# One transpose for a tile's raw queries and keys, with GpSimd splitting them after the turn

## The chip, the cores and the metric

The kernel runs on one core of a Trainium2 chip. The metric is the device time of one execution in microseconds (us). Times of one kernel agree within about 0.03% here (999.93 to 1000.2 us in three runs).

## The reference

Attention with a threshold, then a mixture of experts, then a small network:

```python
scores = scale * q @ k.T                          # 4 x 8 heads, 576 rows, 64 columns, fp32
thresh = max(scores, rows) - tau
attn   = exp(where(scores >= thresh, scores, -1e9) - max)
x      = (attn / (sum(attn) + 1e-9)) @ v          # -> 2304 tokens x 512
x      = gate * relu(x @ w1[expert]) @ w2[expert] # one of 8 experts per token
out    = (h * sigmoid(1.702 h)) @ w_out, h = x @ w_in
```

## The kernel before

Each product of fp32 numbers is made of products of parts in the type float32r: a number is split into a high part (a copy into the type) and a low part (the number less the high part). For the scores, the 64 columns of a head fill only half of the 128 rows of TensorE's array, so the high and low parts of the queries lie one above the other (high in the upper 64 partitions, low in the lower 64) and are multiplied by the keys' parts in the same order and, in a second pass, in the swapped order (`k_swap`). The two passes give all four products.

**Pairs and steps.** Two heads of the same number in two batches make a pair. There are 16 pairs. Their 2 x 576 rows are turned as nine tiles of 128 rows: tiles 0 to 3 are rows of the first head (side 0), tile 4 has the last 64 rows of both, tiles 5 to 8 are the second head (side 1). So a pair has nine steps, u = 0 to 8 (`U`), two pairs make a quad (18 steps, i), and n counts steps over all pairs. Quad 0 is written out, quads 1 to 3 (pairs 2 to 7) are a rolled loop (`Fori`), quads 4 to 7 are written out again (`over_quads`), as other work is set between their steps. Each engine has its own program of the same steps. Nothing but semaphores orders them.

**What the engines do in step n of pair p:**
- TensorE: five transposes of the probabilities of step n - 5 (L1520), and between them the transposes of a tile of the *next* pair (L1534: one for the queries' parts, one for the keys'), both into banks of `pt_ps`; then `score(n)` (L1563: four matmuls of 288 columns, eight in step 4, whose tile belongs to both sides) into one of two buffers `s_ps`. In steps 1 and 5 `values` (L1577, 20 matmuls) of the pair before, in steps 3 and 7 `turn` (L1594 to L1602).
- VectorE: L1091 scales the scores into SBUF and takes the row's minimum (`row_low`); L811 writes results in steps 4 and 8; L802 masks the probabilities of step n - 2 with the threshold.
- GpSimd: L712 makes the threshold of the row from its minimum. Between the thresholds: in step 0 `split(pair + 1, 1)` and in step 5 `split(pair + 2, 0)` (L651 copy, L653 subtract, on the raw tiles `qk` with rows in partitions, into `qk_parts`); in step 1 `swap(pair, j, 1)` and in step 6 `swap(pair + 1, 1 - j, 0)` (L661, L663: two copies of 64 partitions x 576 from `qkT` to `k_swap`, each from one half of the partitions to the other).
- ScalarE: copies the turned probabilities to `pT` (L1302, L1307) and the turned queries and keys to `qkT` (L1315, in step 4 L1311 to L1313), then takes exp of the scores of step n - 1 (L1386). In steps 2 and 6 it copies the values' result (L1371).
- SyncE: loads the next pairs' queries, keys and values (`load_a`, `load_b`, `load_v`) and stores x; `load_a` and `load_b` wait until the split has read the buffer (`parts_ready`).

**The waits around the change.** `score` in step 0 waits for the swap of side 0, in step 4 for that of side 1:

```python
if u == 0:
    wait(pe, k_swapped, (quad * 2 + j) * 4 + 2)
if u == TAIL:
    wait(pe, k_swapped, (quad * 2 + j) * 4 + 4)
...
wait(pe, low_ready, n - 1)
```

The transposes of tile 0 and of tile 5 wait for their side's split. GpSimd takes its instructions in the order of its program, and each threshold waits for L1091 of its step.

After the attention come a mixture of experts on tiles of 256 tokens and the last network. GpSimd gathers the first two blocks of tokens for them in quad 7 (steps i = 3 and 11), and the first expert's weights are loaded to where `qk` lies.

Of the kernel before, what the change touches and what calls it, by code (L numbers as in the profile page):

```python
# [6 lines left out]
ALU = mybir.AluOpType  # L7
# [9 lines left out]
P = 128  # L17


def attention_moe_mlp_kernel(nc, q, k, v, tau, modality_id, w_gate, modality_bias, w1, w2, w_in, w_out, out):  # L20
# [54 lines left out]
    with ctx:  # L75
# [27 lines left out]
        qk = put("qk", [P, U, 2, DH], at=DB * F1)  # L103
        qk_parts = put("qk_parts", [P, U, 2, 2, DH], F32R)
# [3 lines left out]
        qkT = [put(f"qkT{b}", [P, 2, 2 * SPAD], F32R) for b in range(2)]  # L108
# [156 lines left out]
        first_a = [s_ps[0][:, c] for c in range(2)]  # L265
        first_t = [s_ps[1][:, c, 0:P] for c in range(2)]
        first_b = [pt_ps[:, 0:TAIL].rearrange("p a n -> p (a n)"), misc[:]]
# [13 lines left out]
        qk_a_loaded = sem("qk_a_loaded")  # L281
        qk_b_loaded = sem("qk_b_loaded")
        v_loaded = [sem(f"v_loaded{b}") for b in range(2)]
        k_swapped = sem("k_swapped")
        first_parts = sem("first_parts")
# [121 lines left out]

        A_ROWS, T_ROWS, B_ROWS = slice(0, TAIL), slice(TAIL, TAIL + 1), slice(TAIL + 1, U)
# [31 lines left out]
        def _(sp):  # L440
# [6 lines left out]
            def load_a(quad, j):  # L447

                if on(quad, 1, QUADS) or j == 1:
                    if isinstance(quad, int) and quad == 0:  # L450
                        sp.wait_ge(first_parts, 2)
                    else:
                        wait_apart(sp, parts_ready, (quad * 2 + j) * 4 - 4)
                for c, src in enumerate((q_v, k_v)):
                    one, two = seqs_of(src, quad, j)
                    sp.dma_start(qk[:, A_ROWS, c], one[0:SEQ - LAST].rearrange("(t p) d -> p t d", p=P)).then_inc(qk_a_loaded, 16)
                    sp.dma_start(qk[0:LAST, TAIL, c], one[SEQ - LAST:]).then_inc(qk_a_loaded, 16)
                for c, src in enumerate((q_v, k_v)):
                    one, two = seqs_of(src, quad, j)
                    sp.dma_start(qk[LAST:P, TAIL, c], two[SEQ - LAST:]).then_inc(qk_a_loaded, 16)  # L460

            def load_b(quad, j):

                wait_apart(sp, parts_ready, (quad * 2 + j) * 4 - 2)
                one, two = seqs_of(q_v, quad, j)
                for units, at in B_QUERIES:
                    sp.dma_start(qk[:, units, 0], two[at].rearrange("(t p) d -> p t d", p=P)).then_inc(qk_b_loaded, 16)
                one, two = seqs_of(k_v, quad, j)
                sp.dma_start(qk[:, B_ROWS, 1], two[0:SEQ - LAST].rearrange("(t p) d -> p t d", p=P)).then_inc(qk_b_loaded, 16)
# [32 lines left out]
            def load_w1(expert, turn):  # L502
                for a in range(DB):
# [26 lines left out]
            def early_part(quad, j):  # L530
# [6 lines left out]
                if (quad, j) == (QUADS - 2, 1):  # L537
                    sp.wait_ge(first_expert_ready, 1)
                    load_w1(sp.value_load(first_expert_i[0:1], min_val=0, max_val=E - 1), 0)
                if (quad, j) == (QUADS - 1, 1):  # L540
                    sp.wait_ge(turned, UNITS)
                    sp.wait_ge(order_stored, 16)
                    load_w2(sp.value_load(first_expert_i[0:1], min_val=0, max_val=E - 1), 0)

            def step(quad):
                for j in range(2):
                    pair = quad * 2 + j
                    if isinstance(quad, int):
                        early_part(quad, j)
                    if on(pair, 0, PAIRS):  # L550
                        load_v(quad, j)
                    if on(pair, 2, PAIRS + 2):
                        store_x(quad - 1, j)
                    if on(pair, 0, PAIRS - 2):
                        load_b(quad + 1, j)
                    if on(pair, 0, PAIRS - 3):
                        load_a(quad + 1 + j, 1 - j)

            sp.dma_start(qk[:, A_ROWS, 0], q_v[0, 0:SEQ - LAST].rearrange("(t p) d -> p t d", p=P)).then_inc(qk_a_loaded, 16)
# [1275 lines left out]
```

## Time and profile before

| | |
|---|---|
| median of 3 runs | 999.98 us |
| profiled execution | 1000.17 us, span 998.6 us |
| attention stage | from the first score at 11.02 us to about 335 us |
| TensorE busy in the span | 972.2 us (97%) |
| VectorE, ScalarE, GpSimd | 502.7, 447.3, 256.2 us |
| TensorE's mean granted clock | 0.995 |
| chain that ended last | TensorE 92%, VectorE 3% |

Busy time is the union of an engine's instructions. TensorE's matmuls overlap in it, so what one costs is read from the chain of waits, where pieces follow each other. The span is shorter than the execution's own time by 1.57 us.

### The profile page before, as it was taken

What the parts mean: (1) busy time and instruction counts of PE and PEld (TensorE: products, weight loads), DVE (VectorE), ACT (ScalarE), POOL (GpSimd) and SP (SyncE); (2) the same over time, 40 slices, a digit from 0 to 9 for tenths busy, and PEclk for the clock granted to TensorE, in tenths of its full rate; (3) what the DMA queues carried; (4) which work ended last, traced back from release to release, by engine and by line L of the source; (5) the groups of instructions that cost most, each with busy time, mean ns of one, the idle gap of its engine ahead of it and who ended that gap; (6) DMA issues with size and microseconds to landing.
All of it is one profiled execution on the core that took longest, in us unless ns stands there. A gap on an engine that the chain in (4) does not pass through costs nothing.

```text
span 998.6 us, 18965 instructions
## 1 busy us (share of the span) xinstructions
PE 972.2 (97%) x6508; PEld 867.1 (87%) x6509; DVE 502.7 (50%) x1142; ACT 447.3 (45%) x1013; POOL 256.2 (26%) x357
## 2 busy tenths in 40 slices
PE   5999999999999999999999999999999999999996
PEld 5778787878787799999999999989999999999995
DVE  6988788888889685212125155522223223222221
ACT  4778787878788514221124154422222222222221
POOL 5655565556565212111112100010010100100101
PEclk8999999999999999999999999999999999999999
DMA  3323222222344118511112542200100101000000
GB/s 62 73 60 72 47 60 65 66 49 61 91 103 130 38 42 255 178 42 42 42 42 79 173 159 64 64 32 1 32 32 0 56 7 32 32 0 0 32 1 32
DMA packets 106904, 61.08 MB, mean 61 GB/s; under 512 B 87373, under 2 KB 95587, under 8 KB 106851
## 3 DMA queue, kind: packets, MB, share of 16 engines
q1 hardware_dynamic: 96195, 44.36, 16.9%
q0 software_dynamic: 4160, 10.51, 3.4%
q10 hardware_dynamic: 6496, 5.54, 1.7%
q8 instruction: 28, 0.46, 0.2%
q14 instruction: 25, 0.20, 0.1%
HBM read 45.68 MB, written 14.70 MB: 60 GB/s over the span
## 4 chain that ended last, share of the span: by engine, by line
PE 92%; DVE 3%; issue 2%; ACT 1%; POOL 1%; DMA 0%; SPq 0%; ACTq 0%; POOLq 0%; DVEq 0%
PE s_ps L1790 20%; PE s_ps L1762 13%; PE s_ps L1628 11%; PE o_ps L1577 9%; PE pt_ps L1520 9%; PE s_ps L1563 8%; PE pt_ps L1762 6%; PE misc L1710 5%; PE o_ps L1710 5%; PE pt_ps L1534 3%; PE misc L1602 1%; PE pt_ps L1620 1%; PE misc L1594 1%; DMA qk<-in_k_dram 0%; ACT probs L1386 0%
## 5 line engine op out<-in xcount | busy, mean ns | idle before, releaser
L1279 DVE TENSOR_TENSOR g<-s_ps,sig 128x384 f32<-128x384 f32 x96 | 53.5, 557 | 277.1 <-ACT sig L1491 277.1
L1491 ACT ACTIVATE sig<-s_ps 128x384 f32<-128x384 f32 x96 | 47.2, 492 | 271.5 <-PE s_ps L1790 271.5
L1091 DVE TENSOR_SCALAR_CACHE_REDUCE scores<-s_ps,taus 128x576 f32<-128x576 f32 x144 | 117.7, 817 | 47.5 <-PE s_ps L1563 30.2
L802 DVE SCALAR_TENSOR_TENSOR probs<-scores,thresh,probs 128x576 f32<-128x576 f32 x144 | 136.6, 950 | 0.0
L1520 PE MATMUL pt_ps<-ident,probs 128*128 128x128 f32 x720 | 127.0, 278 | 3.9 <-ACT pT L1302 1.8
L1790 PE MATMUL s_ps<-yT_high,w_in_high 128*128 (+1 forms) x384 | 129.5, 337 | 0.3 <-issue 0.2
L1790 PE MATMUL s_ps<-yT_high,w_in_low 128*128 (+1 forms) x384 | 129.5, 337 | 0.0
L1790 PE MATMUL s_ps<-yT_low,w_in_high 128*128 (+1 forms) x384 | 128.9, 336 | 0.0
L757 POOL DMA_INDIRECT out_dram<-out_sb,table x18 | 17.8, 989 | 417.7 <-ACT out_sb L1466 414.7
L1386 ACT ACTIVATE probs<-scores,row_low 128x576 f32<-128x576 f32 x144 | 115.4, 801 | 7.5 <-DVE scores L1091 6.1
L1520 PEld LDWEIGHTS pt_ps<-ident,probs 128*128 128x128 f32 x720 | 83.5, 141 | 28.0 <-issue 18.4
L712 POOL TENSOR_TENSOR thresh<-row_low,taus 128x1 f32<-128x1 f32 x144 | 74.1, 515 | 121.4 <-DVE scores L1091 115.0
L1563 PE MATMUL s_ps<-qkT 128*128 128x288 f32 x320 | 102.2, 336 | 1.8 <-DVE k_swap L796 1.2
L1577 PE MATMUL o_ps<-pT,vv 128*64 128x320 f32 x640 | 93.2, 437 | 0.0
L1628 PE MATMUL s_ps<-xT_high,w_high 128*128 128x256 f32 x320 | 91.3, 285 | 1.8 <-issue 1.0
L1628 PE MATMUL s_ps<-xT_low,w_high 128*128 128x256 f32 x320 | 90.5, 283 | 0.0
L1628 PE MATMUL s_ps<-xT_high,w_low 128*128 128x256 f32 x320 | 90.5, 283 | 0.0
L1563 PE MATMUL s_ps<-k_swap,qkT 128*128 128x288 f32 x320 | 89.7, 296 | 0.0
L1302 ACT COPY pT<-pt_ps 128x512 f32<-128x512 f32 x144 | 85.3, 592 | 7.1 <-PE pt_ps L1520 4.3
L1790 PEld LDWEIGHTS s_ps<-yT_high,w_in_high 128*128 128x128 f32 x384 | 72.2, 188 | 5.1 <-issue 1.1
L1762 PE MATMUL s_ps<-w_out_high,g_low 128*128 128x512 f32 x192 | 76.2, 397 | 0.0
L1762 PE MATMUL s_ps<-w_out_low,g_high 128*128 128x512 f32 x192 | 75.8, 395 | 0.0
(277 smaller groups left out, 2177.7 us busy)
## 6 DMA issues: line engine op xcount, KB each, us to landing
w_raw<-in_moe_w_dram SPq DMA_DIRECT2D x24, 512.0 KB, 4.6
yT_dram<-tile_yT ACTq DMA_DIRECT2D x10, 512.0 KB, 3.0
x_dram<-xs SPq DMA_DIRECT2D x32, 128.0 KB, 2.2
w_in_raw<-in_moe_w_in_dram SPq DMA_DIRECT2D x4, 1024.0 KB, 5.9
w_out_raw<-in_moe_w_out_dram SPq DMA_DIRECT2D x16, 256.0 KB, 2.6
qk<-in_k_dram SPq DMA_DIRECT2D x30, 128.0 KB, 2.4
next_yT<-yT_dram SPq DMA_DIRECT2D x5, 768.0 KB, 4.4
qk<-in_q_dram SPq DMA_DIRECT2D x16, 128.0 KB, 2.1
```

The source lines that it names most:

```text
L712: pool.tensor_tensor(thresh[:, j, u:u + 1], row_low[:, j, u:u + 1], taus[:, 4:5], ALU.add).then_inc(thresh_ready, 1)
L802: dve.scalar_tensor_tensor(out=probs[:, i % PROB_SLOTS, 0:SEQ], in0=scores[:, i % SCORE_SLOTS], scalar=thresh[:, j, u:u + 1], in1=probs[:, ...
L1091: dve.tensor_scalar(scores[:, i % SCORE_SLOTS].rearrange("p (c n) -> p c n", c=2), s_ps[i % 2][:, :, 0:HALF], taus[:, 3:4], None, ALU.mult ...
L1302: act.copy(pT[:, 0:TAIL, v * P:(v + 1) * P], pt_ps[:, 0:TAIL]).then_inc(keys_copied, 1)
L1386: act.activation(probs[:, k % PROB_SLOTS, 0:SEQ], scores[:, k % SCORE_SLOTS], ACT.Exp, bias=row_low[:, k // U, k % U:k % U + 1], scale=-1. ...
L1520: return pe.transpose(pt_ps[:, block], probs[:, k % PROB_SLOTS, block * P:(block + 1) * P], ident[:])
L1563: mm = pe.matmul(s_ps[i % 2][:, c, 0:HALF], qkT[j][:, 0, q_tile * P:(q_tile + 1) * P], keys[:, first:first + HALF], start=(at == 0), stop= ...
L1577: mm = pe.matmul(o_ps[lo:lo + DH, 0:UP], vv[j][:, side, block], pT[:, block, at:at + UP], start=(block == 0), stop=(block == TPB - 1))
L1628: mm = pe.matmul(hT_ps[f // 2][:, f % 2 * T:(f % 2 + 1) * T], w_part[:, a, f * P:(f + 1) * P], x_part[:, a], start=(a == 0 and part == 0), ...
L1710: mm = pe.matmul(yT_ps[d // 2][:, d % 2 * T:(d % 2 + 1) * T], w_part[:, f, d * P:(d + 1) * P], h_part[:, f], start=(at == 0 and part == 0) ...
L1762: mm = pe.matmul(mlp_y_ps[i], g_part[:, f % GT, at], w_part[:, f, :], start=(f == 0 and part == 0), stop=(f == FB2 - 1 and part == 2))
L1790: mm = pe.matmul(mlp_h_ps[f % 2], w_part[:, a, f * P:(f + 1) * P], y_part[:, bass.ds(c % 2 * DB + a, 1)].rearrange("p a b -> p (a b)"), st ...
```

## The change

The raw queries and keys of a tile lie side by side in the 128 columns of `qk` (64 and 64), so that one transpose turns both: queries land in partitions 0 to 63 (`TOP`), keys in 64 to 127 (`BOTTOM`). ScalarE copies the turned raw tiles to `qkT_raw`, two tiles at a time, in steps 1, 3, 4, 6 and 8. GpSimd splits what has been turned, in three groups for each side, each behind the threshold of its step: the keys (high part to the lower half of `k_swap`, low part to the lower half of `k_parts`), copies of both to the upper halves, and the queries. `qk` gets two buffers, which are loaded as soon as they have been turned. The pair's score waits for all three groups of its side. The first pair's parts are made by ScalarE, VectorE and GpSimd together. The early gathers move from steps 3 and 11 of quad 7 to 12 and 14.

GpSimd:

```diff
-            def split(pair, side):
-                tiles = slice(0, TPB) if side == 0 else B_ROWS
...
-                pool.tensor_copy(qk_parts[:, tiles, :, 0], qk[:, tiles]).then_inc(parts_ready, 1)
-                wait(pool, parts_ready, done + 1)
-                pool.tensor_tensor(qk_parts[:, tiles, :, 1], qk[:, tiles], qk_parts[:, tiles, :, 0].bitcast(F32), ALU.subtract
-                                   ).then_inc(parts_ready, 1)
+            def split_keys(pair, j, side):
+                cols = K_COLS[side]
+                done = pair * 8 + side * 4 - 4
+                wait_apart(pool, turned_copied, pair * U + (TPB if side == 0 else U))
+                pool.tensor_copy(k_swap[j][BOTTOM, cols], qkT_raw[BOTTOM, cols]).then_inc(parts_ready, 1)
+                wait_apart(pool, parts_ready, done + 1)
+                pool.tensor_tensor(k_parts[j][BOTTOM, cols], qkT_raw[BOTTOM, cols], k_swap[j][BOTTOM, cols].bitcast(F32),
+                                   ALU.subtract).then_inc(parts_ready, 1)
+                wait_apart(pool, parts_ready, done + 2)
+            def swap_keys(pair, j, side):
...
+                pool.tensor_copy(k_parts[j][TOP, cols], k_swap[j][BOTTOM, cols]).then_inc(k_swapped, 1)
+                wait_apart(pool, k_swapped, done + 1)
+                pool.tensor_copy(k_swap[j][TOP, cols], k_parts[j][BOTTOM, cols]).then_inc(k_swapped, 1)
+                wait_apart(pool, k_swapped, done + 2)
+            def split_queries(pair, j, side):
+                cols, to = K_COLS[side], Q_COLS[side]
+                done = pair * 8 + side * 4 - 2
+                pool.tensor_copy(q_parts[j][TOP, to], qkT_raw[TOP, cols]).then_inc(parts_ready, 1)
+                wait_apart(pool, parts_ready, done + 1)
+                pool.tensor_tensor(q_parts[j][BOTTOM, to], qkT_raw[TOP, cols], q_parts[j][TOP, to].bitcast(F32),
+                                   ALU.subtract).then_inc(parts_ready, 1)
+                wait_apart(pool, parts_ready, done + 2)
...
-                    if u == 0 and on(pair, 0, PAIRS - 1):
-                        split(pair + 1, 1)
...
-                    if u == 1 and on(pair, 0, PAIRS):
+                    if u == 0 and on(pair, 1, PAIRS):
                         wait_apart(pool, thresh_ready, n + 1)
-                        swap(pair, j, 1)
-                    if u == 5 and on(pair, 0, PAIRS - 2):
-                        split(pair + 2, 0)
+                        split_keys(pair, j, 1)
+                    if u == 1 and on(pair, 1, PAIRS):
+                        wait_apart(pool, thresh_ready, n + 1)
+                        swap_keys(pair, j, 1)
+                    if u == 2 and on(pair, 1, PAIRS):
+                        wait_apart(pool, thresh_ready, n + 1)
+                        split_queries(pair, j, 1)
+                    if u == 5 and on(pair, 0, PAIRS - 1):
+                        wait_apart(pool, thresh_ready, n + 1)
+                        split_keys(pair + 1, 1 - j, 0)
                     if u == 6 and on(pair, 0, PAIRS - 1):
                         wait_apart(pool, thresh_ready, n + 1)
-                        swap(pair + 1, 1 - j, 0)
+                        swap_keys(pair + 1, 1 - j, 0)
+                    if u == 7 and on(pair, 0, PAIRS - 1):
+                        wait_apart(pool, thresh_ready, n + 1)
+                        split_queries(pair + 1, 1 - j, 0)
```

ScalarE (in `copy_turned`) and TensorE:

```diff
+        TURN_TILES = {1: (0, 2), 3: (2, 4), 4: (4, 5), 6: (5, 7), 8: (7, 9)}
...
+                if with_qk and tu in TURN_TILES:
+                    if tu in (1, TAIL):
+                        wait(act, parts_ready, pair * 8 + (0 if tu == 1 else 4))
...
+                    last = act.copy(qkT_raw[:, first * P:end * P].rearrange("p (a n) -> p a n", n=P),
+                                    pt_ps[:, QK_AT:QK_AT + end - first])
...
                 if with_qk:
-                    for c in range(2):
-                        mm = pe.transpose(pt_ps[:, QK_AT + c],
-                                          qk_parts[:, tu, c].rearrange("p a d -> p (a d)").bitcast(F32), ident[:])
+                    mm = transpose_qk(1 - j, tu, pt_ps[:, QK_AT + TURN_SLOT[tu]])
...
+                if u in (0, TAIL):
+                    side = 0 if u == 0 else 1
+                    wait(pe, parts_ready, pair * 8 + side * 4)
+                    wait(pe, k_swapped, (pair * 2 + side) * 2)
```

SyncE: `load_a` and `load_b` wait for `turned` instead of `parts_ready`; the order in a step becomes load_b, (w1 in part), load_v, load_a, (rest of w1), store_x:

```diff
+                if on(quad, 1, QUADS):
+                    wait_apart(sp, turned, (quad * 2 + j - 1) * U)
...
+                    if on(pair, 0, PAIRS - 2):
+                        load_b(quad + 1, j)
...
                     if on(pair, 0, PAIRS):
                         load_v(quad, j)
+                    if on(pair, 0, PAIRS - 2):
+                        load_a(quad + 1, j)
...
                     if on(pair, 2, PAIRS + 2):
                         store_x(quad - 1, j)
-                    if on(pair, 0, PAIRS - 2):
-                        load_b(quad + 1, j)
-                    if on(pair, 0, PAIRS - 3):
-                        load_a(quad + 1 + j, 1 - j)
```

## Rows read from the trace of the kernel before

**Rows 1.** Busy time by stretch: PE, PEld, DVE, ACT, POOL, granted clock, DMA share, GB/s.

```profile
50.00:80.00 30.00, 29.90 (x233) 24.19 (x233) 25.31 (x61) 24.05 (x62) 16.77 (x26) 1.00 0.31 70
```

**Rows 2.** The chain of waits in the rolled loop: start, us, what.

```profile
109.24 0.70 PE s_ps L1563 x4
...
110.50 0.22 PE pt_ps L1534 x2
...
110.83 0.52 PE s_ps L1563 x4
111.35 2.84 PE o_ps L1577 x20
...
118.28 1.06 PE s_ps L1563 x8
...
131.31 2.84 PE o_ps L1577 x20
```

**Rows 3.** GpSimd's timeline in the rolled loop: start, us, what, idle before.

```profile
107.01 0.66 POOL L661 CAST k_swap<-qkT 64x576 fp32r<-64x576 f32 x1 [0.26 <-ACT qkT L1315]
107.84 1.20 POOL L663 CAST k_swap<-qkT 64x576 fp32r<-64x576 f32 x1 [0.17 <-POOL k_swap L661]
109.35 0.19 POOL L712 TENSOR_TENSOR thresh<-row_low,taus 128x1 f32<-128x1 f32 x1 [0.32 <-POOL k_swap L663]
...
113.24 1.27 POOL L653 TENSOR_TENSOR qk_parts<-qk,qk_parts 128x512 fp32r<-128x512 f32 x1
```

**Rows 4.** GpSimd's groups by form, 60 to 330 us: busy, mean ns, idle before.

```profile
L663 POOL CAST k_swap<-qkT 64x576 fp32r<-64x576 f32 x26 | 20.4, 784 | 2.8 <-POOL k_swap L661 1.8
...
L653 POOL TENSOR_TENSOR qk_parts<-qk,qk_parts 128x640 fp32r<-128x640 f32 x12 | 18.7, 1555 | 1.0
L653 POOL TENSOR_TENSOR qk_parts<-qk,qk_parts 128x512 fp32r<-128x512 f32 x12 | 15.3, 1274 | 1.0
L651 POOL CAST qk_parts<-qk 128x640 fp32r<-128x640 f32 x12 | 8.6, 718 | 0.0
L651 POOL CAST qk_parts<-qk 128x512 fp32r<-128x512 f32 x12 | 7.3, 605 | 0.0
```

**Rows 5.** VectorE's timeline in the rolled loop.

```profile
106.95 0.82 DVE L1091 TENSOR_SCALAR_CACHE_REDUCE scores<-s_ps,taus 128x576 f32<-128x576 f32 x1 [0.24 <-POOL thresh L712]
...
107.69 0.81 DVE L802 SCALAR_TENSOR_TENSOR probs<-scores,thresh,probs 128x576 f32<-128x576 f32 x1
...
108.76 0.82 DVE L1091 TENSOR_SCALAR_CACHE_REDUCE scores<-s_ps,taus 128x576 f32<-128x576 f32 x1 [0.24 <-DVE probs L802]
...
109.50 0.53 DVE L811 TENSOR_TENSOR xs<-misc,row_inv 128x360 f32 x1
...
113.56 1.57 DVE L802 SCALAR_TENSOR_TENSOR probs<-scores,thresh,probs 128x576 f32<-128x576 f32 x1
```

**Rows 6.** GpSimd's timeline where the steps are written out.

```profile
246.70 0.66 POOL L661 CAST k_swap<-qkT 64x576 fp32r<-64x576 f32 x1
247.42 0.67 POOL L663 CAST k_swap<-qkT 64x576 fp32r<-64x576 f32 x1
248.17 0.58 POOL L712 TENSOR_TENSOR thresh<-row_low,taus 128x1 f32<-128x1 f32 x1
```

**Rows 7.** The timeline of the start, all engines.

```profile
5.39 0.83 DVE L773 TENSOR_TENSOR qk_parts<-qk,qk_parts 128x640 fp32r<-128x640 f32 x1
...
11.02 0.37 PE L1563 MATMUL s_ps<-qkT 128*128 128x288 f32 x1 [1.17 <-DVE k_swap L796]
...
14.97 0.19 POOL L712 TENSOR_TENSOR thresh<-row_low,taus 128x1 f32<-128x1 f32 x1
```

**Rows 8.** SyncE's waits over the span: total us, times, longest.

```profile
SPq L456 <- POOL qk_parts L653: 94.6, 13, 9.4
```

**Rows 9.** Busy time by stretch at the start, columns as in rows 1.

```profile
11.00:13.50 2.50, 0.77 (x4) 0.55 (x4) 0.83 (x2) 0.00 (x0) 2.24 (x3) 0.81 0.45 101
...
17.00:19.00 2.00, 2.00 (x11) 1.97 (x10) 1.21 (x3) 1.59 (x4) 1.76 (x5) 0.50 0.10 19
```

More of the change, by code:

```diff
@@ L107, in attention_moe_mlp_kernel @@
         xs = [put("xs0", [P, U, HEADS, XW], at=3 * DB * F1)]
-        qkT = [put(f"qkT{b}", [P, 2, 2 * SPAD], F32R) for b in range(2)]
+        q_parts = [put(f"q_parts{b}", [P, 2 * SPAD], F32R) for b in range(2)]
+        k_parts = [put(f"k_parts{b}", [P, 2 * SEQ], F32R) for b in range(2)]
         k_swap = [put(f"k_swap{b}", [P, 2 * SEQ], F32R) for b in range(2)]
@@ L656, in swap @@
-            def swap(pair, j, side):
-                wait_apart(pool, turned_copied, pair * U + (TPB if side == 0 else U))
-                cols = slice(side * SEQ, (side + 1) * SEQ)
-                done = pair * 4 + side * 2
-                pool.tensor_copy(k_swap[j][0:DH, cols], qkT[j][DH:P, 1, cols]).then_inc(k_swapped, 1)
+            def split_keys(pair, j, side):
[7 more added lines that the diff above has]
+                wait_apart(pool, parts_ready, done + 2)
@@ L1296, in _, with copy_turned @@
         def _(act):
[L1298 removed]
+            def copy_turned(m, v, pair, tu, with_probs, with_qk, extra=None):
                 if with_probs:
@@ L1551, in score @@
                 j, u = i // U, i % U
-                if u == 0:
-                    wait(pe, k_swapped, (quad * 2 + j) * 4 + 2)
-                if u == TAIL:
-                    wait(pe, k_swapped, (quad * 2 + j) * 4 + 4)
-                sides = ((TAIL, 0), (U, 1)) if u == TAIL else ((u, 0 if u < TAIL else 1),)
-                passes = [(q_tile, side, keys) for q_tile, side in sides for keys in (qkT[j][:, 1], k_swap[j])]
+                pair = quad * 2 + j
+                if isinstance(n, int) and n == 0:
+                    pe.wait_ge(first_queries, 2)
+                    pe.wait_ge(first_keys, 2)
+                    pe.wait_ge(first_swapped, 2)
+                if u in (0, TAIL):
+                    side = 0 if u == 0 else 1
+                    wait(pe, parts_ready, pair * 8 + side * 4)
+                    wait(pe, k_swapped, (pair * 2 + side) * 2)
+                sides = ((TAIL, 0), (TPB, 1)) if u == TAIL else ((u, 0) if u < TAIL else (u + 1, 1),)
+                passes = [(q_tile, side, keys) for q_tile, side in sides for keys in (k_parts[j], k_swap[j])]
                 wait(pe, low_ready, n - 1)
```

185 lines of the change are left out of this document (95 added, 90 removed).

## The prediction

> **What bounds the kernel now.** I read the stretches first, then the chain of waits, then the three engines that feed each other in one pair of heads. In the attention stage (about 11 to 335 us) TensorE is busy 29.90 of 30 us while VectorE has 25.31, ScalarE 24.05 and GpSimd 16.77 [rows 1]. The chain of waits runs on TensorE alone, and one pair of heads takes 131.31 - 111.35 = 19.96 us of it [rows 2]. So GpSimd looks idle for 13 of 30 us. That average is what misleads here, and what the reader is to see is *when* GpSimd works, since the pair's scores wait for it in two places.
>
> A pair has nine steps, u = 0 to 8. The line of instructions that matters is: PE score(u), VectorE L1091 (scores and row minimum, "TS" below, 0.82 us), GpSimd L712 (the threshold), then in some steps a group of GpSimd work, then the next thing that waits for that group. At 107.84 GpSimd starts the last copy of the swapped keys, which ends at 109.04; TensorE's score(0) of the next pair starts within 0.2 us of that (its piece of the chain begins at 109.24), and its piece of the chain is 0.70 us where the plain one is 0.52 [rows 2, 3]. GpSimd is therefore already 0.18 us late at this point, with a load of two groups (split in step 5, swap in step 6). Anything that is put behind them delays score(0).
>
> **The part that gains.** Two transposes of the keys' and queries' parts (0.22 us on the chain for two [rows 2]) become one: 0.11 us x 9 tiles = 0.98 us a pair, over 15 pairs in the loop 14.7 us. This is what a TensorE bound kernel would get, and 999.98 would become about 985.
>
> At this place the Trainium skill, "TensorE: Matmul & The Clock Gate", section "Part 4: PE-mode transpose", gives about 275 ns for one transpose in a kernel. By that as the price, 135 transposes would be worth an estimated 37 us. The chain gives 0.11 us from one to the next because they are pipelined, and the chain decides; neither figure matters if TensorE isn't what sets the pace, which is the case below.
>
> **The part that costs: GpSimd.** Removed per pair: two splits (0.61 + 1.27 and 0.72 + 1.56 us) and four swap copies of 64x576 (0.66 each). Added: for each side, a key split (copy, subtract), two copies to the upper partitions, a query split (copy, subtract). All are 64x576. A copy of this shape is 0.66 us [rows 3]. The subtract of this shape isn't in the trace. A 128x512 one takes 1.274 and a 128x640 one 1.555 [rows 4]; the copy of 64x576 (0.66) is longer than that of 128x512 (0.605 [rows 4]), so the length counts and half the partitions give nothing back. I take 1.41, by length between the two. Bounds: 0.66 (no dearer than a copy) and 1.56. GpSimd's own instructions in a pair, thresholds aside, go from 6.8 to 8 x 0.66 + 4 x 1.41 = 10.9 us. This still fits in 20. The order doesn't:
>
> Work for a side sits in three consecutive steps, each group after that step's threshold, and all three have to be done before TensorE may do score(0) (steps 5, 6, 7) and score(4) (steps 0, 1, 2). Before, the step 5 group wasn't waited for by score(0), and step 7 had none.
>
> A first bound needs nothing of the groups before: step 7's query split can't start until TS(7) has ended. In the trace TS(7) starts at 106.95, ends at 107.77, and score(0) starts by 109.2 [rows 2, 5]. Threshold 0.19, gap 0.30, copy 0.66, gap 0.17, subtract 1.41 and 0.13 for a semaphore from engine to engine ("hop", an estimate between the gaps of 0.06 in rows 6 and 0.17 in rows 3) give 107.9 + 2.9 = 110.8. That is 1.6 us late even with GpSimd free, and TensorE has no slack: against 0.49 us saved per half pair. The same holds for score(4).
>
> The full loop, for pairs 2 to 7 (the rolled loop over quads). Gaps on GpSimd there, from rows 3: threshold end to copy 0.26 (taken 0.30, since two waits stand there now); copy to copy 0.17; last copy to the next threshold 0.31 (taken 0.29).
> - Half one, from the end of score(0): hop 0.13, TS(0) 0.82, the threshold behind the mask that starts at once (0.81 and an estimated 0.05) = 1.8; key split 0.30 + 0.66 + 0.17 + 1.41 + 0.29 = 2.8; threshold 0.2; copies up 0.30 + 0.66 + 0.17 + 0.66 + 0.29 = 2.1; threshold 0.2; query split 0.30 + 0.66 + 0.17 + 1.41 = 2.5; hop 0.1. Together 9.8 us until score(4) may start.
> - Half two: score(4) 1.06 (eight matmuls [rows 2]), hop 0.15, TS(4) 0.82, L811 0.45 to 0.53, mask 0.81, gap 0.24, TS(5) 0.82, threshold behind its mask 0.86 = 5.3; the three groups 7.8; hop 0.1; score(0) 0.5 = 13.7 us.
> - Sum 23.5 us. To this come holds between VectorE's mask (L802) and GpSimd. Rows 3 and 5 show both directions: the copy at 107.84 takes 1.20 instead of 0.66 since the mask beside it runs from 107.69, and the mask at 113.56 takes 1.57 instead of 0.81 because GpSimd's subtract holds from 113.24 to 114.51. A copy's mean is 784 ns against 660 [rows 4], so 0.12 each for 12 instructions and an estimated 0.15 each for the four thresholds left: 2.0 us. Period 25.5 us, that is +5.5.
>
> The pairs outside the rolled loop (0, 1 and 8 to 15) have gaps of only 0.06 and 0.08 us [rows 6]. Eight gaps a half fall from 2.0 to about 0.56 us, so 2.9 us less a pair: 22.6 us, +2.7.
>
> Six pairs at +5.5 and, counted by groups run (half of pair 0, pairs 1 and 8 to 14, half of pair 15), nine at +2.7: 33 + 24.3 = **57.3 us**. TensorE's own work is 19.96 - 0.98 = 19.0 us a pair, so in this state it idles 6.5 us a pair in the rolled loop, some 3.3 before each of score(0) and score(4), and 1.8 before each outside it; its saving of 14.7 us lies inside that idle time and is worth nothing.
>
> **What is free.** The start: VectorE's split ahead of the first transposes goes (the subtract alone 0.83 us), five transposes fewer and other copies make the first score start about 1.4 us sooner than 11.02. But GpSimd now has six instructions for side 1 ahead of its constants, so its first threshold comes some 1.5 us later than 14.97 [rows 7]. I count zero, between -1.5 and +1.5. ScalarE's copies of turned tiles fall from eleven to five a pair; it is busy 24 of 30 us, off the path, so no gain; it too now waits for GpSimd in steps 1 and 4, but for the same groups as TensorE. Its exp queued behind that wait feeds a mask two steps later, which the stalled scores delay anyway. DMAs: the same loads, into two buffers, waiting for the transposes instead of the split; SP waited 94.6 us in 13 times for the old split [rows 8], so its queue has room for loads of w1 set between them and for stores behind them. The two gathers move behind the last groups, into steps 3 and 5 of the last pair; nothing but thresholds with two steps of slack stands behind them.
>
> Sum on the profiled execution: 1000.17 + 57.3 = 1057.5 us; it lies 0.19 above the median of 999.98, so 1057.
>
> **Rivals.**
> - *GpSimd's chain as above* (0.66): 1057, between 1027 (no holds, 2 us a pair less: 6 x 3.5 + 9 x 0.7) and 1066 (the subtract at 1.56, 0.6 us a pair more).
> - *The clock joins in* (0.18). At the start TensorE is busy 0.77 of 2.5 us [rows 9], the granted clock falls to 0.81 in the mean, and is then 0.50 (1.2 GHz) while the engine is busy 2.00 of 2.00. The idle stretches of some 3.3 us that I expect in the rolled loop are longer than that whole stretch of idle time (2.50 - 0.77). Each would make the following values (2.84 us) and scores up to twice as long. Their delay is partly in the idle time that follows; I count 1 us for each half in the rolled loop and 0.5 outside, 12 + 9 = 21 us: 1078; with 2 us for every half, 1117. In the trace of before nothing idles for so long in a loop, so how often the clock falls is open. The Trainium skill has the rule on the page "TensorE: Matmul & The Clock Gate", section "Why this matters for your kernels": idle gaps between bursts of matmuls put the array back on half its clock. By that rule the stalls of the rolled loop would trigger it.
> - *The subtract of 64 partitions is cheap* (0.10). At 0.66 to 0.8 us each half is 1.2 to 1.5 us shorter: the rolled pairs get 22.5 to 23.0 and the others 19.6 to 20.2, hence 6 x 2.8 + 9 x 0 = +17: about 1017. Against it: rows 4, where length alone counts.
> - *TensorE sets the pace, the groups are hidden* (0.03), the other sign: 985. It needs step 7's group to be done 1.6 us sooner than the earliest possible end worked out above, on both sides of the pair. It decides at a group (copy and subtract with gaps) of 1.2 us or less, less than two plain copies. For it speaks only GpSimd's low share.
> - *Savings and stalls cancel* (0.03): subtract near 0.7 and no holds: about 1000.
>
> **Numbers.** The likeliest gives 1057. With 2 in 10 left out, the range reaches down past part of the cheap subtract and up into the clock case: 1030 to 1088. A difference of 0.2% (2 us) is about what can be told from no change here. Slower 0.94, within 0.2% 0.02, faster 0.04.
>
> **What the profile would show.** Attention stage longer, the rest the same; values (L1577's successor) 25 us apart in the rolled loop from one pair to the next and 22 to 23 after it; TensorE waiting for GpSimd's second query subtract ahead of score(0) and score(4), some 3 us in the rolled loop; VectorE waiting for TensorE's scores far more than before; the chain of waits passing through GpSimd; subtracts of 64x576 near 1.41 us; GpSimd's busy time up by some 4 us a pair. I'd be wrong if the subtract is much below 1.3, if the masks give way less often, or, upwards, if the granted clock in 50 to 170 us is well under 1.

## The result and the profile after

The median is 1084.07 us (1083.87 to 1084.54 in four runs) against 999.95 us of the kernel before on the same chip: a ratio of 1.0841, 95% interval [1.0823, 1.086], slower by 84 us. The forecast was 1057 in a range of 1030 to 1088.

The waits of the new kernel, 20 to 400 us (engine, line, releaser: us in total, times, longest). L1608 is the score, L682 the query split's subtract, L735 the threshold, L1120 TS (the scaling with the row's minimum):

```profile
POOL thresh L735 <- DVE scores L1120: 92.5, 53, 2.6
DVE scores L1120 <- PE s_ps L1608: 91.4, 67, 3.2
...
PE s_ps L1608 <- POOL q_parts L682: 62.1, 29, 3.5
```

The same stretch in the kernel before, where L1091 is TS, L1563 the score and L663 the last copy of the swap:

```profile
DVE scores L1091 <- PE s_ps L1563: 24.9, 27, 1.9
PE s_ps L1563 <- POOL k_swap L663: 0.5, 1, 0.5
```

It is a circle: VectorE waits for scores, GpSimd for VectorE, TensorE for GpSimd's last instruction. 29 waits are two for each pair, score(0) and score(4), as forecast. In 60 to 180 us GpSimd has at least 35% of the chain of waits; before, TensorE had all but 0.2% of it.

GpSimd's timeline in one rolled pair, which answers to [rows 3]:

```profile
167.84 0.62 POOL L735 TENSOR_TENSOR thresh<-row_low,taus 128x1 f32<-128x1 f32 x1 [2.35 <-DVE scores L1120]
168.80 0.66 POOL L661 CAST k_swap<-qkT_raw 64x576 fp32r<-64x576 f32 x1 [0.34 <-ACT qkT_raw L1346]
169.65 1.40 POOL L663 TENSOR_TENSOR k_parts<-qkT_raw,k_swap 64x576 fp32r<-64x576 f32 x1 [0.18 <-POOL k_swap L661]
...
175.11 0.61 POOL L735 TENSOR_TENSOR thresh<-row_low,taus 128x1 f32<-128x1 f32 x1 [1.75 <-DVE scores L1120]
175.89 0.66 POOL L680 CAST q_parts<-qkT_raw 64x576 fp32r<-64x576 f32 x1 [0.17 <-POOL thresh L735]
176.73 1.39 POOL L682 TENSOR_TENSOR q_parts<-qkT_raw,q_parts 64x576 fp32r<-64x576 f32 x1 [0.18 <-POOL q_parts L680]
...
182.97 0.62 POOL L735 TENSOR_TENSOR thresh<-row_low,taus 128x1 f32<-128x1 f32 x1 [1.98 <-DVE scores L1120]
...
190.65 1.69 POOL L682 TENSOR_TENSOR q_parts<-qkT_raw,q_parts 64x576 fp32r<-64x576 f32 x1 [0.18 <-POOL q_parts L680]
```

and TensorE's, in the same stretch:

```profile
178.35 0.39 PE L1608 MATMUL s_ps<-k_parts,q_parts 128*128 128x288 f32 x1 [1.83 <-POOL q_parts L682]
...
192.56 0.60 PE L1608 MATMUL s_ps<-k_parts,q_parts 128*128 128x288 f32 x1 [3.37 <-POOL q_parts L682]
192.96 0.44 PE L1608 MATMUL s_ps<-k_swap,q_parts 128*128 128x288 f32 x1
```

The subtract at 176.73 ends at 178.12, score(4) starts at 178.35; the one at 190.65 ends at 192.34, score(0) starts at 192.56. Query splits stand behind thresholds that themselves wait for VectorE (1.75 us at 175.11). And the second matmul after the long stall takes 0.44 us, not the 0.29 of full clock. The stretches around it (columns as in [rows 1]) say why:

```profile
188.00:190.00 2.00, 1.16 (x9) 0.72 (x7) 1.76 (x5) 2.00 (x7) 1.51 (x3) 1.00 0.31 69
190.00:192.00 2.00, 0.00 (x0) 0.00 (x0) 1.09 (x3) 0.62 (x1) 1.82 (x2) 0.82 0.64 144
192.00:194.00 2.00, 1.44 (x6) 1.43 (x7) 0.00 (x0) 0.00 (x0) 0.53 (x2) 0.50 0.29 65
194.00:196.00 2.00, 2.00 (x10) 1.78 (x8) 1.56 (x4) 1.22 (x4) 0.65 (x2) 0.50 0.61 139
```

TensorE idles, the granted clock falls to 0.50 (1.2 GHz), and the scores and values that all others wait for run on it: in step 1 the values of 20 matmuls cost up to 3.91 us in the chain of waits instead of 2.84 [rows 2]. In 60 to 180 us the granted clock is 0.89 in the mean. The Trainium skill's "TensorE: Matmul & The Clock Gate", section "Why this matters for your kernels", says that an idle gap between bursts of matmuls puts the array back on half its clock; the trace agrees (0.50 behind the 3.37 us).

```profile
60.00:180.00 120.00, 96.60 (x642) 73.93 (x641) 77.25 (x177) 65.21 (x150) 68.87 (x94) 0.89 0.21 46
```

GpSimd's groups by form, 40 to 400 us (busy us, mean ns):

```profile
L682 POOL TENSOR_TENSOR q_parts<-qkT_raw,q_parts 64x576 fp32r<-64x576 f32 x29 | 42.2, 1456 | 3.5 <-POOL q_parts L680 2.2
L663 POOL TENSOR_TENSOR k_parts<-qkT_raw,k_swap 64x576 fp32r<-64x576 f32 x28 | 39.9, 1425 | 3.4 <-POOL k_swap L661 2.2
```

**Where the 84 us lie.** TensorE's `values` in step 1 of a pair is a good milestone. For pairs 1, 2, 8 and for the last values but one (step 1 behind pair 15, "16"), first before, then after:

```profile
31.35 2.91 PE L1577 MATMUL o_ps<-pT,vv 128*64 128x320 f32 x20
51.31 2.91 PE L1577 MATMUL o_ps<-pT,vv 128*64 128x320 f32 x20
171.19 2.91 PE L1577 MATMUL o_ps<-pT,vv 128*64 128x320 f32 x20
331.44 2.91 PE L1577 MATMUL o_ps<-pT,vv 128*64 128x320 f32 x20
```

```profile
35.44 4.00 PE L1622 MATMUL o_ps<-pT,vv 128*64 128x320 f32 x20
60.52 3.42 PE L1622 MATMUL o_ps<-pT,vv 128*64 128x320 f32 x20
223.20 3.99 PE L1622 MATMUL o_ps<-pT,vv 128*64 128x320 f32 x20
415.18 2.91 PE L1622 MATMUL o_ps<-pT,vv 128*64 128x320 f32 x20 [1.47 <-DMA vv<-in_v_dram]
```

| stretch | before | after | more | forecast |
|---|---|---|---|---|
| start to pair 1 | 31.35 | 35.44 | +4.1 | 0 and half a pair, 1.35 |
| pair 1 | 19.96 | 25.08 | +5.1 | +2.7 |
| pairs 2 to 7, rolled | 119.88 | 162.68 | +42.8 (27.1 each) | +33 (25.5 each) |
| pairs 8 to 15 | 160.25 | 191.98 | +31.7 (24.0 each) | +20.25 |

These sum to 83.7 of the 84; what follows the attention is unchanged.

### The profile page after: what moved, and what is told of

Its sections match the earlier page's. It is cut to its first block, busy times and chain, and to the rows that moved or that the text cites. A ratio compares the mean times of both kernels' runs of the same rounds, so it can differ in the third digit from the quotient of the medians.

```text
span 1082.5 us, 18734 instructions
## 1 busy us (share of the span) xinstructions
PE 989.1 (91%) x6364; PEld 870.1 (80%) x6365; DVE 524.6 (48%) x1138; ACT 430.9 (40%) x922; POOL 325.5 (30%) x420
## 4 chain that ended last, share of the span: by engine, by line
PE 74%; POOL 10%; issue 6%; DVE 6%; ACT 1%; DMA 1%; POOLq 1%; SPq 0%; DVEq 0%; ACTq 0%
PE s_ps L1828 18%; PE s_ps L1800 12%; PE s_ps L1673 10%; PE o_ps L1622 7%; PE pt_ps L1800 6%; PE s_ps L1608 6%; PE misc L1748 5%; PE o_ps L1748 5%; POOL q_parts L682 4%; PE pt_ps L1561 3%; DVE probs L831 2%; POOL thresh L735 1%; DVE scores L1120 1%; POOL k_parts L663 1%; POOL q_parts L680 1%
## 5 line engine op out<-in xcount | busy, mean ns | idle before, releaser
L1608 PE MATMUL s_ps<-k_parts,q_parts 128*128 128x288 f32 x320 | 110.1, 359 | 69.8 <-POOL q_parts L682 64.7
L1120 DVE TENSOR_SCALAR_CACHE_REDUCE scores<-s_ps,taus 128x576 f32<-128x576 f32 x144 | 117.7, 817 | 105.5 <-PE s_ps L1608 95.6
L831 DVE SCALAR_TENSOR_TENSOR probs<-scores,thresh,probs 128x576 f32<-128x576 f32 x144 | 156.1, 1085 | 1.2 <-POOL thresh L735 1.2
L1608 PEld LDWEIGHTS s_ps<-k_parts,q_parts 128*128 128x128 f32 x320 | 66.5, 208 | 77.6 <-POOL q_parts L682 38.5
L1561 PEld LDWEIGHTS pt_ps<-ident,probs 128*128 128x128 f32 x720 | 89.2, 147 | 31.1 <-issue 20.8
L735 POOL TENSOR_TENSOR thresh<-row_low,taus 128x1 f32<-128x1 f32 x144 | 71.3, 496 | 123.0 <-DVE scores L1120 96.5
L1622 PE MATMUL o_ps<-pT,vv 128*64 128x320 f32 x640 | 101.8, 468 | 1.5 <-DMA vv<-in_v_dram 1.5
L1608 PE MATMUL s_ps<-k_swap,q_parts 128*128 128x288 f32 x320 | 96.4, 316 | 0.0
L1622 PEld LDWEIGHTS o_ps<-pT,vv 128*64 128x64 f32 x640 | 46.5, 149 | 45.3 <-issue 13.6
```

The source lines that it names most:

```text
L735: pool.tensor_tensor(thresh[:, j, u:u + 1], row_low[:, j, u:u + 1], taus[:, 4:5], ALU.add).then_inc(thresh_ready, 1)
L831: dve.scalar_tensor_tensor(out=probs[:, i % PROB_SLOTS, 0:SEQ], in0=scores[:, i % SCORE_SLOTS], scalar=thresh[:, j, u:u + 1], in1=probs[:, ...
L1120: dve.tensor_scalar(scores[:, i % SCORE_SLOTS].rearrange("p (c n) -> p c n", c=2), s_ps[i % 2][:, :, 0:HALF], taus[:, 3:4], None, ALU.mult ...
L1561: return pe.transpose(pt_ps[:, block], probs[:, k % PROB_SLOTS, block * P:(block + 1) * P], ident[:])
L1608: mm = pe.matmul(s_ps[i % 2][:, c, 0:HALF], q_parts[j][:, q_tile * P:(q_tile + 1) * P], keys[:, first:first + HALF], start=(at == 0), stop ...
L1622: mm = pe.matmul(o_ps[lo:lo + DH, 0:UP], vv[j][:, side, block], pT[:, block, at:at + UP], start=(block == 0), stop=(block == TPB - 1))
```

## The experiments

A table at the end of this part has the milestones for the runs that matter.

**1. The query split made shorter.** The queries' low parts of pairs 2 to 15 are computed for 8 of 576 columns; the rest is left out.

```diff
+                if not (isinstance(pair, int) and pair < 2):
+                    cols, to = slice(cols.start, cols.start + 8), slice(to.start, to.start + 8)
                 pool.tensor_tensor(q_parts[j][BOTTOM, to], qkT_raw[TOP, cols], q_parts[j][TOP, to].bitcast(F32),
                                    ALU.subtract).then_inc(parts_ready, 1)
```

> The changed kernel, with the queries' low part made in full for the first two pairs only; for the 14 others the subtract runs on 8 of 576 columns (the scores then use stale low parts). Theory (the chain through GpSimd's groups sets the pace): each of the 28 sides loses about 1.25 us of the chain, so 1084 - 35 = 1049 us, and some 5 to 10 us more if the granted clock recovers with shorter stalls (1040 to 1050). Rival, TensorE sets the pace: 1084, no change. Rival, the masks held up by GpSimd set it: 28 holds of up to 0.8 us go, 1084 - 20 = 1064, with TensorE's waits for GpSimd as long as before.

Measured 1042.94 us, 1.0426 [1.0408, 1.0443]; TensorE's waits for this instruction 33.0 us (25 times) instead of 62.1, granted clock in 60 to 180 us 0.93 instead of 0.89. The last instruction of the third group is on the path. The subtract's mean falls from 1.46 to 0.28 us, 1.18 us less, which is 33 us for 28 of them; 41 us come back. The other 8 us fit what the expectation gave for a recovering clock (5 to 10 us), but this run does not show them apart. The rival of the masks, with TensorE's waits as long as before, is refuted by those waits.

**2. The transposes of raw tiles issued twice.**

```diff
-                    mm = transpose_qk(1 - j, tu, pt_ps[:, QK_AT + TURN_SLOT[tu]])
+                    for again in range(2):
+                        mm = transpose_qk(1 - j, tu, pt_ps[:, QK_AT + TURN_SLOT[tu]])
```

> The changed kernel, with each transpose of a raw tile done twice into the same place, as many transposes as before the change. Theory (TensorE's saving lies inside its own idle time): 1084 to 1092, the upper end because with the clock down the steps after score(0) are on the path too. Rival (TensorE's saving was banked and is part of the result): 135 x 0.11 = 15 us more, 1099.

Measured 1081.13 us, 1.0814 [1.0793, 1.0836]. The whole saving of the change on TensorE, given back, costs nothing; the median is even 3 us lower, below what either theory gave (the two intervals overlap a little). The granted clock is 0.91 instead of 0.89 in 60 to 180 us, which may be the reason; no run tests it apart.

**3. The clock held up.** Before its wait ahead of score(0) and score(4), from step 9 on, TensorE transposes the identity into the score's free bank.

```diff
                 if u in (0, TAIL):
                     side = 0 if u == 0 else 1
+                    if not isinstance(n, int) or n > U:
+                        wait(pe, low_ready, n - 1)
+                        for filler in range(26 if u == 0 and not isinstance(n, int) else 14):
+                            pe.transpose(s_ps[i % 2][:, 0, 0:P], ident[:], ident[:])
                     wait(pe, parts_ready, pair * 8 + side * 4)
```

> The changed kernel, with transposes of the identity into the scores' bank just ahead of TensorE's wait for GpSimd: 26 (about 2.9 us) ahead of score(0) in the rolled loop, 14 (1.5 us) elsewhere. Theory (after a stall the clock is down, and values of 3.9 us instead of 2.84 delay the third threshold of the group): granted clock back to 1.00, 20 values of 2.84 us, the rolled pair 27.3 -> 25.5 to 26 us, the others -0.7: about 1069. Rival (the chain through GpSimd alone makes the period, the clock is paid inside the stall): 1084 within 3 us, though the clock is up. Against both: more than 1090 would mean that the fillers themselves are on the path.

Measured 1066.49 us, 1.0664 [1.0646, 1.0682]. Stretches and waits of this run:

```profile
60.00:180.00 120.00, 110.57 (x857) 89.85 (x854) 76.50 (x186) 68.57 (x160) 73.19 (x98) 1.00 0.20 45
```

```profile
159.90 0.37 PE L1612 MATMUL s_ps<-k_parts,q_parts 128*128 128x288 f32 x1 [0.62 <-POOL q_parts L682]
...
171.78 0.37 PE L1612 MATMUL s_ps<-k_parts,q_parts 128*128 128x288 f32 x1 [1.70 <-POOL q_parts L682]
```

The clock is 1.00 although TensorE still has to wait for GpSimd after the fillers, so they delay no score here; of the 30 scores that follow a query subtract, one starts late (0.73 us behind it, at 57.1 us, the others 0.05 to 0.25). The clock's share is 1084.07 - 1066.49 = 17.6 us; the other 66.5 us are there at full clock.

GpSimd's timeline shows where the clock had entered GpSimd's chain. In the changed kernel the threshold of step 2 stood idle for TS (1.75 us at 175.11), whose score comes behind the slow values of step 1. Here it follows the copies at once:

```profile
168.57 0.19 POOL L735 TENSOR_TENSOR thresh<-row_low,taus 128x1 f32<-128x1 f32 x1 [0.32 <-POOL k_swap L673]
```

From score(0) to score(4) the rolled pair takes 11.9 us here (159.90 to 171.78), and 13.1 in the changed kernel (165.23 to 178.35). The way from score(4) to score(0) is 14.2 us in both.

**4. All six operations of a side behind one threshold**, in steps 0 and 5.

```diff
                     if u == 0 and on(pair, 1, PAIRS):
                         wait_apart(pool, thresh_ready, n + 1)
                         split_keys(pair, j, 1)
-                    if u == 1 and on(pair, 1, PAIRS):
-                        wait_apart(pool, thresh_ready, n + 1)
                         swap_keys(pair, j, 1)
-                    if u == 2 and on(pair, 1, PAIRS):
-                        wait_apart(pool, thresh_ready, n + 1)
                         split_queries(pair, j, 1)
```

> The changed kernel, with all six instructions of a side behind one threshold (steps 5 and 0) instead of in three groups behind three. Theory: threshold to last subtract falls from 9.4 and 10.3 us to 7.2 in the rolled loop and from 9.8 and 8.2 to 6.6 elsewhere, 1084 - 6 x 5.3 - 9 x 4.8 = about 1010 (1003 to 1025), still slower than before the change in the rolled loop. Rival (GpSimd's amount of work or its hold on VectorE's masks is the matter, not its order): 1075 to 1084. Rival: the thresholds of steps 1 and 2, 6 and 7 come too late and the masks wait for them: 1040 or more, with VectorE idle on the threshold.

Measured 1056.96 us, 1.0561 [1.0544, 1.0579]: a gain of 27 us, but far from 1010. The rival of the late thresholds (1040 or more) is in GpSimd's timeline:

```profile
175.11 1.40 POOL L682 TENSOR_TENSOR q_parts<-qkT_raw,q_parts 64x576 fp32r<-64x576 f32 x1 [0.18 <-POOL q_parts L680]
176.82 1.16 POOL L735 TENSOR_TENSOR thresh<-row_low,taus 128x1 f32<-128x1 f32 x3 [0.32 <-POOL q_parts L682]
```

Three thresholds come in a row behind the group that began at 169.56, and VectorE's masks wait for them (10.8 us in 8 times in 60 to 180 us). So placing the groups together trades some late scores for late thresholds; TensorE's waits for the query split are still 45.8 us (25 times, 20 to 400 us).

**5. The high parts made by ScalarE** straight from PSUM, so that GpSimd has two subtracts and two copies for a side, in one group.

```diff
+                    here, of = slice(first * P, end * P), pt_ps[:, QK_AT:QK_AT + end - first]
+                    act.copy(k_swap[1 - j][BOTTOM, here].rearrange("p (a n) -> p a n", n=P), of[BOTTOM])
...
+                        act.copy(q_parts[1 - j][TOP, first * P + shift:end * P + shift].rearrange("p (a n) -> p a n", n=P),
+                                 of[TOP])
+                    last = act.copy(qkT_raw[:, here].rearrange("p (a n) -> p a n", n=P), of)
```

> The changed kernel, with ScalarE writing the high parts straight from PSUM (two more copies for each copy of turned tiles) and GpSimd left with two subtracts and two copies up, in one group behind one threshold. The result of the run before it was 1057 (one group of six): threshold to last instruction 7.2 us in the rolled loop, and masks that waited for late thresholds. Theory (length of the group between a threshold and the scores, and how late it makes the next thresholds): the group is 5 us, rolled pairs 24.2 -> 20.5 us, the others near 20.5: about 1005 (990 to 1020). Rival (ScalarE becomes the bound: ten copies of 0.27 us a pair more on 15 of 20 us): 1020 or more, with VectorE and TensorE waiting for ScalarE.

Measured 1026.54 us, 1.0265 [1.0248, 1.0282], outside what the theory gave: the granted clock is 1.00 and TensorE waits for GpSimd once (0.6 us), but it waits 18.5 us (50 times, 20 to 400 us) for ScalarE's copy of raw tiles. ScalarE is busy 99.25 of 120 us (65.21 in the changed kernel, 95.37 in the one before). The time is that of the ScalarE rival, 1020 and more; that it is the cause is read from these waits, as TensorE still has 60% of the chain of waits.

**6. The thresholds moved to ScalarE**, ahead of its exp; GpSimd's groups wait for turned tiles alone.

```diff
+                        act.activation(thresh[:, k // U, k % U:k % U + 1], row_low[:, k // U, k % U:k % U + 1],
+                                       ACT.Identity, bias=taus[:, 4:5], scale=1.0).then_inc(thresh_ready, 1)
                         act.activation(probs[:, k % PROB_SLOTS, 0:SEQ], scores[:, k % SCORE_SLOTS], ACT.Exp,
...
-                        pool.tensor_tensor(thresh[:, j, u:u + 1], row_low[:, j, u:u + 1], taus[:, 4:5], ALU.add
-                                           ).then_inc(thresh_ready, 1)
```

> The changed kernel, with the thresholds (128x1) made by ScalarE ahead of each exp, and GpSimd's six instructions of a side in a row, released by the turned tiles alone. Theory (what cost the time is that the groups stand behind thresholds and thresholds behind groups; the amount of GpSimd's work fits): 6 to 7 us after step 4 or 8 each side is done, before its score; TensorE has no wait for GpSimd, granted clock 1.00, 19.0 to 19.5 us a pair, 985 to 995: faster than before the change. Rival (VectorE, its masks held by 11 us of GpSimd's work a pair, sets the pace at about 20 to 20.5 us): 1000 to 1010, TensorE waiting for VectorE or ScalarE. Rival (GpSimd's amount of work): 1040 or more.

Measured 1007.11 us, 1.0072 [1.0055, 1.0088]. The scores wait for GpSimd's parts only once (0.2 us, 20 to 400 us), and 77 of the 84 us are gone, but not to the 985 to 995 of the theory. The chain of 60 to 180 us has VectorE's mask (L817) at its head, 33%, with "issue" 29%, and the mask is long (VectorE's groups by form, 60 to 180 us):

```profile
L817 DVE SCALAR_TENSOR_TENSOR probs<-scores,thresh,probs 128x576 f32<-128x576 f32 x55 | 61.4, 1116 | 0.0
```

**7. Both moves, 5 and 6 together.**

> Both of the two before: thresholds and high parts on ScalarE, two subtracts and two copies a side on GpSimd. If VectorE's masks are what is left after the thresholds have moved, this is faster than the run with the thresholds alone by some 0.3 us a pair, 5 us (980 to 990). If ScalarE is (2.7 us of copies a pair more), it is slower than that one: 1000 or more.

Measured 1030.48 us, 1.0303 [1.0285, 1.032]: ScalarE is busy 103.98 of 120 us and has 42% of the chain of waits, as much as TensorE (41%); it is slower than run 6, as the ScalarE case of the expectation had it.

**8. The control: the kernel before with its thresholds on ScalarE.**

> Control: the kernel before the change, with the thresholds made by ScalarE; GpSimd still waits for each step's row minimum, and does its splits and swaps as before. Theory (TensorE sets the pace there and GpSimd is late by 0.2 us a pair at most): 996 to 1001. Rival (moving the thresholds is a gain of its own, whatever the transposes): 985 to 992.

Measured 1006.96 us, 1.0067 [1.005, 1.0084], where 996 to 1001 were expected: moving the thresholds costs 7 us by itself (0.36 us of ScalarE each, busy 100.81 of 120 us, and 22% of the chain of waits where it had none before). GpSimd's swaps wait for the splits in this run, as it has no thresholds. Run 6 is to be read against this one: with the thresholds out of GpSimd's way the change is worth 1007.11 - 1006.96, nothing either way.

**9. Each group ahead of its step's threshold** instead of behind it, thresholds on GpSimd.

```diff
+                    if u == 2 and on(pair, 1, PAIRS):
+                        wait_apart(pool, thresh_ready, n)
+                        split_queries(pair, j, 1)
...
                     if on(n, 0, UNITS):
                         wait(pool, low_ready, n + 1)
...
-                    if u == 2 and on(pair, 1, PAIRS):
-                        wait_apart(pool, thresh_ready, n + 1)
-                        split_queries(pair, j, 1)
```

> The changed kernel with each of GpSimd's six groups issued ahead of the threshold of its own step instead of behind it, everything else unchanged. Theory (the groups start too late because each stands behind a threshold, and score(0) and score(4) then wait for the query split): the last group moves one threshold sooner, about 2.3 to 2.5 us in a rolled pair, against stalls of TensorE of 1.83 us before score(4) and 3.37 us before score(0); most of the wait and, with it, most of the half clock should be gone: 1000 to 1020 us, a rolled pair of 20.0 to 21.5 us instead of 27.3, TensorE's waits for the query split under 20 us in sum, granted clock 0.99 or more. Rival (GpSimd's length of work and what it does to VectorE, not its place, sets the time): a threshold is now late by a group of 2.1 us or more, VectorE and ScalarE wait for it, and the time stays at 1040 or above with VectorE's waits for thresholds in the trace.

Measured 1035.12 us, 1.0365 [1.0344, 1.0387]: 49 us come back by a change of order alone (with the clock that came back by it, 0.97 for 0.89), which confirms that the groups stood too late, but the size was missed (1000 to 1020 expected). TensorE's waits for the query split are still 30.9 us. The waits and GpSimd's timeline of this run:

```profile
ACT probs L1421 <- DVE scores L1120: 55.2, 56, 2.1
...
PE s_ps L1608 <- POOL q_parts L682: 30.9, 27, 2.3
```

```profile
181.59 0.35 POOL L753 TENSOR_TENSOR thresh<-row_low,taus 128x1 f32<-128x1 f32 x1 [0.32 <-POOL k_parts L663]
182.10 0.66 POOL L671 CAST k_parts<-k_swap 64x576 fp32r<-64x576 f32 x1 [0.17 <-POOL thresh L753]
182.93 1.27 POOL L673 CAST k_swap<-k_parts 64x576 fp32r<-64x576 f32 x1 [0.17 <-POOL k_parts L671]
184.52 0.19 POOL L753 TENSOR_TENSOR thresh<-row_low,taus 128x1 f32<-128x1 f32 x1 [0.32 <-POOL k_swap L673]
184.88 1.10 POOL L680 CAST q_parts<-qkT_raw 64x576 fp32r<-64x576 f32 x1 [0.17 <-POOL thresh L753]
186.16 1.41 POOL L682 TENSOR_TENSOR q_parts<-qkT_raw,q_parts 64x576 fp32r<-64x576 f32 x1 [0.18 <-POOL q_parts L680]
```

Between instructions only semaphore gaps are left, 0.17 to 0.32 us each. From the first key copy at 178.76 to the last subtract's end at 187.57 GpSimd has no other pause, 8.8 us for one side, in a pair of 22.0 us here. Its busy time in 60 to 180 us is 82.89 of 120; of the other 37.1 us only 14.7 are thresholds waiting for TS, and most of the rest are such gaps.

**10. The same with 8 filler transposes** before score(0) and score(4).

> The run with the groups ahead of their thresholds, and in addition 8 filler transposes of the identity into the free score bank ahead of TensorE's wait before score(0) and score(4) from step 9 on. Theory: where the groups are no longer late the clock is already full and the fillers are worth nothing or cost up to 8 x 0.11 us a half (0.9 us x 30 = 26 us at most, where nothing hides them): within 1% of the run without them. Rival (a stall and a half clock are left): 5 to 15 us faster than the run without fillers, with its clock below 0.99.

Measured 1032.96 us, 1.0333 [1.0317, 1.0349], clock 1.00 instead of 0.97 in 60 to 180 us: 2.2 us less by the medians, with overlapping intervals, and within 1%, as the theory had it. This is the clock's worth less the fillers' own cost: eight of 30 scores now start 0.4 to 1.4 us behind their query subtract (two in run 9), an estimated 6 us in all. The rest of run 9's loss is not the clock: at 1.00 the kernel is still 33 us above the one before.

**11. Run 6 without the subtracts.** Both low parts, of queries and keys, are computed for 8 of 576 columns in pairs 2 to 15; the rest is left out.

> The run with the thresholds on ScalarE (1007.1 us), and in addition GpSimd's two low-part subtracts cut from 576 to 8 columns for pairs 2 to 15, so the low parts of queries and keys are left out there. Theory (with TensorE no longer waiting for GpSimd, what holds that run at the control's 1007 is VectorE, whose masks are held to 1.1 to 1.8 us while GpSimd's subtracts run beside them): masks fall back to a mean under 0.9 us, VectorE's busy time in 60:180 from 107.4 to under 98 of 120 us, and the time to 990 to 1000 us. Rival (ScalarE with its thresholds, or SyncE and the waits between engines, holds that run): masks get shorter but the time stays at 1003 to 1008.

Measured 994.47 us, 0.9947 [0.9934, 0.9961]. VectorE's groups by form and the stretch 60 to 180 us:

```profile
L821 DVE SCALAR_TENSOR_TENSOR probs<-scores,thresh,probs 128x576 f32<-128x576 f32 x56 | 50.6, 904 | 0.0
```

```profile
60.00:180.00 120.00, 117.51 (x885) 91.56 (x881) 97.95 (x246) 96.47 (x261) 46.65 (x75) 1.00 0.27 60
```

The mask's mean falls from 1116 to 904 ns, the time by 12.6 us, and TensorE leads the chain again (30% values, 20% and 17% transposes and scores). ScalarE is as busy as in run 6 (96.47 and 97.70 of 120 us), so its rival is out. What held run 6 was VectorE, held in turn by GpSimd's subtracts beside it.

The milestones, us for each pair:

| run | first values | pairs 2 to 7 | pairs 8 to 15 | time |
|---|---|---|---|---|
| before | 31.35 | 19.98 | 20.0 | 999.95 |
| after | 35.44 | 27.1 | 24.0 | 1084.07 |
| 3, clock held | 35.41 | 25.8 | 23.05 | 1066.49 |
| 9, groups first | 32.78 | 22.6 | 22.1 | 1035.12 |
| 6, thresholds on ScalarE | 30.81 | 20.2 | 20.6 | 1007.11 |
| 8, its control | 31.35 | 20.3 | 20.6 | 1006.96 |
| 11, no subtracts | 30.35 | 19.6 | 19.8 | 994.47 |

No run that computes everything beats the kernel before.

## Why the prediction was right, and where its sizes were off

- **Mechanism: right.** TensorE waits for the second query subtract ahead of score(0) and score(4) (29 times), VectorE for scores, the rest of the kernel is unchanged, and the subtract of 64x576 has a mean of 1.43 to 1.46 us for the 1.41 taken. The cheap subtract is refuted: no half price for half the partitions.
- **TensorE's saving is worth nothing: right** (run 2). Something like it appears only where GpSimd no longer weighs on anyone: a rolled pair of 19.59 us in run 11 against 20.34 of the control (run 8), 0.75 us for the 0.98 worked out. This is no clean measure of it, for run 11 also lacks the subtracts and has fewer copies on ScalarE.
- **Rolled pair: 25.5 forecast, 25.8 with the clock held** (run 3). The sum of groups, gaps and holds was good to 0.3 us. By halves, start of score to start of score and with 1.0 us of holds in each, it gave 11.3 us from score(0) to score(4) (9.8 + 0.5 + 1.0) and 14.2 us back; run 3 has 11.9 and 14.2.
- **Pairs outside: 22.6 forecast, 23.05 with the clock held.** One term shown too small: a threshold there was taken at 0.2 us and a gap of 0.07, but from its start to the copy behind it are 0.64 us (242.26 to 242.90):

```profile
242.26 0.58 POOL L735 TENSOR_TENSOR thresh<-row_low,taus 128x1 f32<-128x1 f32 x1
242.90 0.66 POOL L680 CAST q_parts<-qkT_raw 64x576 fp32r<-64x576 f32 x1
```

  The short gap was read from rows 6 without the long threshold beside it (0.58 at 248.17 [rows 6]). For the four such thresholds of a pair this is 1.5 us, more than the 0.45 us missed, so something else was counted too high; no run shows what.
- **Start: counted zero, measured 4.1 us to the first values**, of which 1.35 were in the sum. The first score comes at 12.00, a microsecond later, not 1.4 sooner, for VectorE's first subtract takes 1.84 us beside GpSimd's; the first threshold comes at 18.36 against 14.97 [rows 7] where 1.5 later was said. That fits the late first values: in run 6, whose thresholds don't queue behind GpSimd's first six operations, they come at 30.81.
- **The clock: this is the step that failed.** It was set apart as a rival of 0.18 with 21 us, and 1057 left it out. It was worth 17.6 us (run 3), and came in where the forecast took step 2's threshold as ready: that threshold waited 1.75 us for a score behind values at half clock, so that score(0) to score(4) took 13.1 us instead of 11.3, while the other half was met (14.2). My own idle of 3.3 us before score(0) (3.37 measured) already exceeded the idle stretch at the start at which the clock had fallen [rows 9]; the two belonged in one case, 1078.

The sum as measured: GpSimd's chain and the start 66.5 us (57.3 forecast), clock 17.6. Of the 9 us between the two, the start has 2.7 us, pair 1 1.0, the six rolled pairs 1.9 and pairs 8 to 15 3.9. The result lies inside the range because the range was drawn to reach into the clock case; the likeliest value, 1057, did not hold it.

What stays open: whether the doubled transposes truly gain 3 us and by what, and how the last 3.9 us divide between the hold of masks and the thresholds' length.

## What to carry to other kernels

An engine that is idle for half of the time may have no room at all at the place that counts: lay its instructions, with the semaphore gaps and what each stands behind, between the event that releases the first and the one that waits for the last. Work that several engines hand around in a circle belongs ahead of short, urgent instructions only as far as those can wait: a change of order was worth 49 us here, the clock included. When a forecast makes TensorE idle for some microseconds in every round, price the half clock into the same case.

## What the runs showed of the hardware

- Transposes as fillers kept the granted clock at 1.00 (run 3), where the same loop without them has 0.89.
- A stall of 1.84 us before score(0) at 245.10 was followed by a clock of 0.50 (247 to 249 us), one of 1.34 us at 256.74 by 1.00 throughout. But so was the one of 1.83 us before score(4) at 178.35: the stall's length alone does not tell.

```profile
178.00:180.00 2.00, 1.65 (x13) 1.65 (x14) 0.94 (x3) 0.94 (x2) 0.47 (x2) 1.00 0.00 0
...
247.00:249.00 2.00, 2.00 (x9) 1.21 (x9) 1.44 (x5) 1.38 (x4) 1.86 (x3) 0.50 0.32 68
...
257.00:259.00 2.00, 2.00 (x18) 2.00 (x17) 1.35 (x6) 1.07 (x2) 0.35 (x1) 1.00 0.00 0
```

- VectorE's mask and GpSimd's subtract hold each other: the mask took 1.98 us instead of 0.81 at 169.69, beside the subtract at 169.65, and the subtract 1.69 instead of 1.39 at 190.65, beside the mask at 190.05. "GPSIMD Engine Reference" of the Trainium skill, section "1. Specifications", has the two engines share an interface to SBUF, with contention for VectorE's instructions with two SBUF inputs; the mask is one, and run 11 agrees (its mean falls from 1116 to 904 ns). TS, which reads the scores from PSUM, has a mean of 818 ns in both.
- An addition of 128x1 on ScalarE takes 0.31 us (run 6) to 0.36 us (run 8) in the mean; nine a pair are 2.8 to 3.3 us of an engine that has little room.
